# The token product as seven block products over sums of its operands

## The reference

```
x = attention(q, k, v)                     # [2, 768, 512]
theta = x @ w_theta
zr, zi = x * cos(theta), x * sin(theta)
y = w_tok_r @ zr + w_tok_i @ zi            # over the 768 tokens, both batches
u = x + y
v = u + relu(u @ w_ch)
h = relu(v @ w_in)                         # [.., 1024]
out = (h * sigmoid(conv3(h))) @ w_out
```

## Time and profile before

| | |
|---|---|
| median of 3 runs | 413.3 us (412.4 to 413.7) |
| the profiled execution's time | 412.85 us |
| its span, first to last instruction | 411.1 us |
| TensorE busy | 404.7 us (98%) |
| VectorE, ScalarE, GpSimd busy | 214.4, 215.9, 129.9 us |
| granted TensorE clock | 1.00 in all forty slices |
| moved by DMA | 32.17 MB |

### The profile page before, as it was taken

One profiled execution on the slowest core, in us unless ns is written; L12 is line 12 of the kernel. 1 busy time (PEld: TensorE's weight loads), 2 busy tenths in 40 slices (PEclk: granted clock), 3 DMA queues, 4 the chain that ended last, 5 costly groups with the idle time before them and its releaser, 6 DMA issues.

```text
span 411.1 us, 6208 instructions
## 1 busy us (share of the span) xinstructions
PE 404.7 (98%) x2268; PEld 349.0 (85%) x2268; DVE 214.4 (52%) x577; ACT 215.9 (53%) x414; POOL 129.9 (32%) x106
## 2 busy tenths in 40 slices
PE   7999999999999999999999999999999999999996
PEld 3888888888788788888898888999999898999985
DVE  5866666665788734537453251477543443434320
ACT  3766666674778546564342320378563635544431
POOL 2293000000266722248412410147653221212120
PEclk9999999999999999999999999999999999999999
DMA  7954442340000322333530000202100200010022
GB/s 253 416 217 158 159 143 93 82 153 4 0 1 2 102 78 77 85 141 125 186 129 1 2 0 0 104 0 53 51 2 0 78 1 1 16 63 2 0 77 77
DMA packets 12271, 32.17 MB, mean 78 GB/s; under 512 B 4176, under 2 KB 4432, under 8 KB 12240
## 3 DMA queue, kind: packets, MB, share of 16 engines
q1 hardware_dynamic: 12240, 31.77, 22.6%
HBM read 28.62 MB, written 3.15 MB: 77 GB/s over the span
## 4 chain that ended last, share of the span: by engine, by line
PE 95%; DVE 2%; issue 2%; ACT 1%; ACTq 0%
PE bank L452 30%; PE bank L591 24%; PE bank L649 16%; PE bank L498 9%; PE bank L470 6%; PE bank L483 6%; PE bank L605 1%; PE bank L562 1%; PE bank L509 1%; DVE xT L1022 0%; ACT trig L776 0%; DVE bank L1030 0%; DVE trig L1129 0%; ACT xT L725 0%; ACT trig L772 0%
## 5 line engine op out<-in xcount | busy, mean ns | idle before, releaser
L591 PE MATMUL bank<-z,wT 128*128 128x512 f32 x432 | 99.3, 390 | 0.0
L591 PEld LDWEIGHTS bank<-z,wT 128*128 128x128 f32 x432 | 80.8, 188 | 16.6
L452 PE MATMUL bank<-vT,win 128*128 128x386 f32 x384 | 73.3, 340 | 0.0
L452 PEld LDWEIGHTS bank<-vT,win 128*128 128x128 f32 x384 | 68.4, 188 | 1.8
L649 PE MATMUL bank<-wout,g 128*128 128x512 f32 x288 | 69.6, 390 | 0.0
L649 PEld LDWEIGHTS bank<-wout,g 128*128 128x128 f32 x288 | 53.9, 188 | 9.7
L1206 DVE SCALAR_TENSOR_TENSOR bank<-h_sb,convw,bank 128x384 f32<-128x384 f32 x32 | 19.9, 623 | 66.7 <-ACT bank L865 66.7
L859 ACT ACTIVATE h_sb<-bank 128x386 f32<-128x386 f32 x32 | 15.8, 494 | 74.0 <-PE bank L452 72.9
L414 POOL TENSOR_TENSOR g<-gf,g 128x384 fp32r<-128x384 f32 x32 | 32.5, 1017 | 68.0 <-ACT g L879 68.0
L498 PE MATMUL bank<-v_sb,pT 128*128 128x65 f32 x352 | 44.6, 268 | 0.0
L498 PEld LDWEIGHTS bank<-v_sb,pT 128*128 128x128 f32 x352 | 43.1, 192 | 0.0
(11 more groups left out here) (77 smaller groups left out, 501.8 us busy)
## 6 DMA issues: line engine op xcount, KB each, us to landing
wrows<-w_tok_laid SPq DMA_DIRECT2D x12, 768.0 KB, 4.4
v_sb<-v_laid SPq DMA_DIRECT2D x8, 780.0 KB, 4.6
qk_sb<-qk_laid SPq DMA_DIRECT2D x7, 792.0 KB, 4.3
out<-ob SPq DMA_DIRECT2D x12, 256.0 KB, 2.2
winraw<-w_in_in SPq DMA_DIRECT2D x4, 512.0 KB, 3.8
woutraw<-w_out_in SPq DMA_DIRECT2D x8, 256.0 KB, 2.7
wthraw<-w_theta_in SPq DMA_DIRECT2D x1, 1024.0 KB, 12.1
wchraw<-w_ch_in SPq DMA_DIRECT2D x1, 1024.0 KB, 5.1
```

What stands on the lines that cost most here:

```text
L452: last = pe.matmul(dst, w[a], m[b], start=(i == 0 and j == 0), stop=(i == n - 1 and j == 2))
L591: last = pe.matmul(Y_BANK[s % 2][:], wT[s % 2][:, hi, ri * NT + blk, :], z[b][:, blk, lo, ri, :], start=(blk == 0 and ri == 0 and j == 0), ...
```

## The change

The product y = [Wr Wi] [zr; zi] for both batches at once is a 2 x 2 block product: the rows of W in two halves of 384, the contraction in the real and the imaginary half (768 each), the columns in two batches of 512. It is now computed by seven block products in place of eight. A block product k is three row tiles i, so s = 3k + i runs from 0 to 20, with 18 matmuls each. The left operands are sums or differences of four blocks of W, the right ones of zr and zi of the two batches (`B_RAW`), and each result is added to or subtracted from one or two chunks of x (`ADDS`).

- Left operands: during attention GpSimd (`prepare`) forms them from the raw weights. Six (k = 0 and 1) stay in SBUF, fifteen go by four staging tiles to DRAM (`store_a`) and come back before their product (`load_a`). Nine of these are stored unsplit and split on return (`high_a` on ScalarE, `low_a` on VectorE, 768 elements). The two buffers of values (v) of attention become three, so that v of a pair is loaded earlier.
- Right operands: z is kept unsplit. `high_b`/`low_b` split one operand of 6 blocks into one of two buffers, in three pieces of 1024 elements. Six differences (three of batch 0, three mixed) are made by VectorE (`own_difference`, `other_difference`), nine sums by GpSimd (`sums`, `last_sums`), 1024 elements each.
- The first block product fills three banks at once, block by block of z, the second the next three; later ones use two banks.
- `add_y` has two VectorE additions for k < 5, one for k = 5 and 6.
- `high_u` writes a second, unrounded copy of u, with which `add_mix` is one VectorE operation in place of two.
- The chunks are finished in the order 1, 2, 0, 3, and the orders of all engines follow that. Loads of w_in and w_out come later.

In the lists of ScalarE and VectorE the lines of the old order that have no part in the new one are left out below.

```diff
--- before.py
+++ after.py
...
+        a_ops = at("a_ops", [P, 6, 2, NT, P], F32R, 41)
...
+        NI = NT // 2
+        NS = 7 * NI
+        NK = 5 * NI
+        ADDS = (((1, ALU.add), (3, ALU.subtract)), ((1, ALU.add), (0, ALU.add)), ((2, ALU.add), (0, ALU.subtract)),
+                ((2, ALU.add), (3, ALU.add)), ((0, ALU.add), (3, ALU.add)), ((0, ALU.add),), ((3, ALU.add),))
+        B_RAW = (zi[0], zi[1], zd, zr[0], zi[0], zr[1])
+        MIXED = (1, 2, 0, 3)
+        U_DONE = (2 * NI, 4 * NI, 6 * NI, 7 * NI)
+
+        def y_bank(s):
+            return bank[(6, 7, 4, 5, 0, 1)[s]] if s < 2 * NI else bank[6 + s % 2]
+
+        def b_side(k):
+            return (k + 1) % 2
...
             def load_v(p):
...
+                if p >= 3:
+                    sp.wait_ge(o_ready, NT * (p - 2))
+                sp.dma_start(v_of[p % 3], v_laid[p]).then_inc(v_in[p % 3], 16)
+
+            def load_w_raw(i):
+                if i >= 2:
+                    sp.wait_ge(staged, 5 * (i - 1))
+                for half in range(2):
+                    sp.dma_start(w_raw[:, i % 2, half].rearrange("p r n -> p (r n)"),
+                                 w_tok[i + NI * half].rearrange("p n c -> p (n c)")).then_inc(w_raw_in[i % 2], 16)
+
+            def store_a(m):
+                i, part = divmod(m, 5)
+                sp.wait_ge(staged, m + 1)
+                whole = slice(0, 2) if part < 2 else slice(0, 1)
+                sp.dma_start(a_kept[NI * part + i][:, whole], stage[m % 4][:, whole].bitcast(F32)).then_inc(stored_a[m % 4], 16)
 
             def banded():
-                for p in range(2, NP):
-                    if p + 1 < NP:
-                        load_qk(p + 1)
+                kept = 0
+                for p, count in zip(range(3, NP), (0, 5, 1, 4, 5)):
+                    load_qk(p)
                     load_v(p)
+                    for m in range(kept, kept + count):
+                        store_a(m)
+                        if m == 4:
+                            load_w_raw(2)
+                    kept += count
...
+            def load_a(n):
+                if n == 0:
+                    for m in range(4):
+                        sp.wait_ge(stored_a[m], 16 * ((NK + 3 - m) // 4))
+                sp.wait_ge(y_ready, n + 1 if n < 4 else n + 3)
...
+            def prepare(i):
+                (w_r0, w_i0), (w_r1, w_i1) = ([w_raw[:, i % 2, half, ri] for ri in range(2)] for half in range(2))
+                pool.wait_ge(w_raw_in[i % 2], 32 * (i // 2 + 1))
+                steps = 7 * i
+
+                def step(ins):
+                    nonlocal steps
+                    ins.then_inc(prep_step, 1)
+                    steps += 1
+                    pool.wait_ge(prep_step, steps)
+
+                def whole(dst, a):
+                    step(pool.tensor_copy(dst[0], a))
+                    return pool.tensor_tensor(dst[1], a, dst[0].bitcast(F32), ALU.subtract)
+
+                def summed(dst, a, b, op):
+                    step(pool.tensor_tensor(w_sum[:], a, b, op))
+                    return whole(dst, w_sum[:])
+
+                def kept(part):
+                    m = 5 * i + part
+                    if m >= 4:
+                        pool.wait_ge(stored_a[m % 4], 16 * (m // 4))
...
+                    return [stage[m % 4][:, half] for half in range(2)]
+
+                def resident(slot):
+                    return [a_ops[:, slot, half].rearrange("p n c -> p (n c)") for half in range(2)]
+
+                if i:
+                    pool.wait_ge(staged, 5 * i)
+                step(summed(resident(i), w_r1, w_i1, ALU.add))
+                whole(resident(NI + i), w_i1)
+                summed(kept(0), w_r0, w_i0, ALU.add).then_inc(staged, 1)
+                whole(kept(1), w_r0).then_inc(staged, 1)
+                for part, a, b, op in ((2, w_r0, w_i1, ALU.add), (3, w_i0, w_i1, ALU.subtract), (4, w_r1, w_r0, ALU.subtract)):
+                    pool.tensor_tensor(kept(part)[0].bitcast(F32), a, b, op).then_inc(staged, 1)
 
             def banded():
                 pool.wait_ge(bias_ready, H)
+                prepare(0)
+                prepare(1)
                 split_w_theta()
-                for s in range(2):
-                    split_rows(s)
+                prepare(2)
...
+            def sums(two):
+                blks = slice(2 * two, 2 * two + 2)
+                for dst, a in ((zr[1], zr[0]), (zr[0], zi[1])):
+                    pool.tensor_tensor(dst[:, blks, :], a[:, blks, :], dst[:, blks, :], ALU.add).then_inc(sum_ready, 1)
+
+            def last_sums(two):
+                blks = slice(2 * two, 2 * two + 2)
+                pool.wait_ge(sum_ready, 2 * two + 2)
+                pool.tensor_tensor(zi[0][:, blks, :], zr[0][:, blks, :], zi[0][:, blks, :], ALU.add).then_inc(sum_ready, 1)
+
+            pool.wait_ge(z_lo, NT)
+            pool.wait_ge(t_ready, NI)
+            sums(0)
+            sums(1)
+            low_v(0)
+            low_v(1)
+            sums(2)
+            low_v(2)
+            pool.wait_ge(b_lo, NI)
+            for two in range(NI):
+                last_sums(two)
+            for n in range(3, 2 * CB):
+                low_v(n)
...
+            def first_tokens():
+                pe.wait_ge(x_done, NU)
+                pe.wait_ge(staged, NK)
+                for blk in range(NT):
+                    pe.wait_ge(z_lo, blk + 1)
+                    for i in range(NI):
+                        for j, (hi, lo) in enumerate(((0, 0), (0, 1), (1, 0))):
+                            last = pe.matmul(y_bank(i)[:], a_ops[:, i, hi, blk, :], b_ops[:, b_side(0), blk, lo, :],
+                                             start=(blk == 0 and j == 0), stop=(blk == NT - 1 and j == 2))
+                        if blk == NT - 1:
+                            last.then_inc(y_ready, 1)
+
             def mix_tokens(s):
...
+                k, i = divmod(s, NI)
+                side, slot = b_side(k), a_slot(s)
+                if k >= 2:
+                    n = s - 2 * NI
+                    if n < 2 * NI:
+                        pe.wait_ge(a_in[n % 4], 16 * (n // 4 + 1))
+                    else:
+                        pe.wait_ge(a_lo, n - 2 * NI + 1)
+                    pe.wait_ge(u_ready, n + 1 if n < 2 else s - 1)
+                for blk in range(NT):
+                    if k >= 1 and i == 0 and blk % 2 == 0:
+                        pe.wait_ge(b_lo, NI * (k - 1) + blk // 2 + 1)
+                    for j, (hi, lo) in enumerate(((0, 0), (0, 1), (1, 0))):
+                        last = pe.matmul(y_bank(s)[:], a_ops[:, slot, hi, blk, :], b_ops[:, side, blk, lo, :],
+                                         start=(blk == 0 and j == 0), stop=(blk == NT - 1 and j == 2))
+                last.then_inc(y_ready, 1)
...
+            first_tokens()
+            for s in range(NI, 2 * NI + 1):
                 mix_tokens(s)
             transpose_u(0)
-            mix_tokens(6)
+            mix_tokens(7)
             mix_channels(0, 0)
             mix_channels(0, 1)
-            mix_tokens(7)
+            mix_tokens(8)
             mix_channels(0, 2)
             mix_channels(0, 3)
+            for s in range(9, 13):
+                mix_tokens(s)
             transpose_u(1)
-            mix_tokens(8)
+            mix_tokens(13)
             mix_channels(1, 0)
             mix_channels(1, 1)
-            mix_tokens(9)
+            mix_tokens(14)
             mix_channels(1, 2)
             mix_channels(1, 3)
+            for s in range(15, 19):
+                mix_tokens(s)
             transpose_u(2)
-            mix_tokens(10)
-            mix_tokens(11)
-            mix_channels(2, 0)
+            mix_tokens(19)
+            for j in range(CB):
+                mix_channels(2, j)
+            mix_tokens(20)
             hidden(0)
-            mix_channels(2, 1)
             transpose_u(3, (0, 1))
             hidden(1)
-            mix_channels(2, 2)
+            transpose_u(3, (2, 3))
             hidden(2)
-            mix_channels(2, 3)
             hidden(3)
-            hidden(4)
-            transpose_u(3, (2, 3))
-            for j in range(CB):
-                hidden(5 + j)
-                mix_channels(3, j)
+            mix_channels(3, 0)
+            mix_channels(3, 1)
+            mix_channels(3, 2)
+            mix_channels(3, 3)
+            for n in range(4, FB + 1):
+                hidden(n)
...
+                if t == 0:
+                    act.wait_ge(staged, NK)
+                    for m in range(4):
+                        act.wait_ge(stored_a[m], 16 * ((NK + 3 - m) // 4))
...
+            def high_b(k):
+                if k >= 2:
+                    act.wait_ge(y_ready, NI * (k - 1))
+                if k == 2:
+                    act.wait_ge(zf_ready, TT)
+                if k == 3:
+                    act.wait_ge(t_ready, NI)
+                if k == 4:
+                    act.wait_ge(sum_ready, 2 * NI)
```

(134 more changed lines are left out.)

315 lines of the change are left out of this document (128 added, 187 removed).

## The result

The changed kernel takes 416.18 us (median of 5 runs, 415.18 to 416.95) against 413.02 (5 runs, 412.4 to 413.7): ratio 1.0074, 95% interval 1.0053 to 1.0095. It is slower by 0.7%. The time lies inside the range and on the wrong side: 412.2 was forecast, with 0.52 for faster. The range held it only because it reached into the case of the falling clock, which had a chance of 0.10.

What follows compares the result with a forecast made beforehand. TensorE, busy for 98% of the span, was taken to bound the kernel. 412.85 - 12.3 (matmuls) - 0.5 (theta) + 12.2 (new waits) = 412.25, forecast 412.2 us, range 405 to 417.5.

Steps and rivals of the forecast that it cites:

- the case of the falling clock: Rival: TensorE's clock falls to 1.2 GHz behind new token-product gaps, net some +5, 417 us; chance 0.10 including a longer backlog.
- -12.3 for 54 matmuls: Token product: 432 matmuls become 378 at 0.228 us each, saving 12.3 us; called the certain part.
- Attention, cost 0: Attention: GpSimd's weight preparation ends near 83 us with slack about 14 us, so nothing reaches TensorE; cost 0.
- Theta, -0.5: Theta stage: splitting z over 512 columns, not 1024, removes a VectorE delay on the chain: -0.5 us (bounds 0 and -1.3).
- How the engines hold each other up: Token product: two-SBUF-input VectorE passes and GpSimd passes exclude each other and alternate, subtractions about 3.3 us; chance 0.62 with the walk's waits.
- VectorE keeps the ports: Rival, token product: VectorE's back-to-back passes hold off a waiting GpSimd; waits 8.1 us, 408.2 us; chance 0.20.
- little of it is felt: Rival, token product: own differences uncontested, sums mostly in VectorE's gaps; waits 3 to 4 us, 403.5 us; chance 0.08.
- The walk: Queues followed by durations around the token product and hidden stage: TensorE waits summing to 12.6 us, taken as 12.2.
- The step that failed: Token product: TensorE's clock taken as 1.00 in the main case, so waits of 2.8 and 4.4 us bring no slowdown.
- the 1.2 forecast ahead of (1,0): After product 12, channel product (1,0) waits for VectorE's low_u(1), at 217.4 against 216.2: 1.2 us.
- the hidden stage, 0.9: Hidden products without channel products between them: two banks absorb most of the 2.97 us step, cost 0.9 us (bounds 0 and 7.8).
- the race of `low_b(4,0)`: At 193.5 us, whether VectorE's low_b(4,0) or GpSimd's sum starts first hangs on 0.15 us, worth 0.8 at product 12.

Runs made afterwards that it cites:

- e7_fill_late: Changed kernel with 17 matmuls that nobody reads filling TensorE's wait ahead of product 12 only: 414.14 us, ratio 1.0039.
- e1_fill: Changed kernel with three TensorE waits of the token product filled by matmuls that nobody reads (12, 4 and 17): 414.49 us, ratio 1.004.
- e6_order3: Changed kernel with VectorE reordered in three parts, the last moving three add_y ahead of low_b(2) and add_mix(12) ahead of hidden 3's convolution: 406.7 us, ratio 0.9858.
- The first two new orders: Changed kernel with VectorE's order altered so additions precede held-up subtractions: first part 412.71 us, second part on top of it 409.14 us.
- the third: Same run as e6_order3, on top of the first two new orders: 406.7 us, ratio 0.9858.
- e4_hidden: Changed kernel with the last four channel products put between hidden products 3 to 8 again, other engines' orders matched: 418.16 us, ratio 1.0124.
- e3_order: Changed kernel, VectorE reordered: add_mix(0), add_mix(1) between the low_b(3); low_a(6), add_y(10) ahead of low_b(4,1), low_b(4,2): 412.71 us, ratio 0.9988.
- e9_halves: e6_order3 with each of GpSimd's nine block sums done as two passes of 512 elements in place of one of 1024: 408.87 us, ratio 0.9888.

## Why the prediction was right and wrong

- **-12.3 for 54 matmuls: right.** L701 and L681 issue 378, and a product takes 4.12 us.
- **Attention, cost 0: right, with a miss on the way.** GpSimd began at 21.9 (it waited for its weights, not for the bias) and ended at 90.6, not 83, 11 us ahead of `turns(0)`, which waits for it. TensorE issued 84 and 83 matmuls in the windows of the earlier trace rows.
- **Theta, -0.5: not shown.** By the same timeline product 0 started at 137.19 in before, at 137.11 in after and at 136.31 to 137.48 in the other profiled runs, which have the same theta stage; that spread is larger than the term.
- **How the engines hold each other up: right.** Alternation pass by pass, 3.3 us a subtraction, is what the timelines show; "VectorE keeps the ports" (408.2) fell at once with the 9.69 us, and "little of it is felt" with it.
- **The walk: right to 0.3 us.** I had `add_mix(0)` end at 184.4, product 12 start at 206.7; the trace has 184.6 and 206.73. The single waits differ (none ahead of product 11, where I had 1.4), because the slow clock had made products 9 and 10 late, and that is the same time put elsewhere: e7_fill_late, where the clock stayed up there, has 1.1 ahead of product 11.
- **The step that failed: that TensorE runs at full clock behind the new waits.** I had taken 1.00 from a trace without such waits, and gave the fall of the clock, with its backlog, 0.10. It fell behind both. What it cost is less than the two slow stretches are long (1.6 and 2.5 us): the first is swallowed by the wait for product 12, the second took the place of the 1.2 forecast ahead of (1,0). The runs put the whole at 1.4 to 1.7 (e1_fill). My "one product each, up to +8, net +5" in the rival was too large in every part but had the place right. It is not enough for the wrong side: e1_fill, with the clock at 1.00, is at 1.004 where the forecast was at 0.9985 of the kernel before, 2.3 us more; the next term and the 0.9 below it make 2.5.
- **The term that was mis-sized: the hidden stage, 0.9.** From hidden product 0 to the first output product it took 31.17 us for 28.7 of matmuls, so 2.5. What it has over the forecast is `add_mix(12)`, which stood behind the convolution of hidden 3. e6_order3 moved it, and the stage took 29.69 us, so 1.0 over the matmuls, close to my 0.9. My walk had put the table load and the copies of u there and not this place in VectorE's order.

From 410.5 (the forecast in terms of the span) to 414.7: +0.9 until product 12 (the theta gain and 0.4 for the race of `low_b(4,0)`, neither of which came), +2.5 for the slow product 12, -1.2 for the wait that it replaced, +1.6 in the hidden stage; 0.4 is left, some 0.02 in each product and 0.15 behind the first output. The chances were wrong as a whole: with the likeliest case at the bound of "same", a term that could only lengthen (the clock) was kept out of it and put in a rival of its own, though the walk itself forecast the waits of 2.8 and 4.4 us.

On the clock, the Trainium skill's rule (page "TensorE: Matmul & The Clock Gate", "Part 1: The HAM clock gate"), that it follows how busy the engine has lately been and has two levels, agrees with the windows at 0.61 and 0.71 behind the waits and with 1.00 once they were filled. On the ports, the Trainium skill's rule (page "SBUF — State Buffer", "SBUF: two separate sides"), that of a VectorE operation with two SBUF inputs and a GpSimd one the first gets the shared ports for its whole instruction, agrees with 3.2 us a subtraction beside the sums and 1.2 without.

## What to carry to other kernels

Where TensorE is the bound, taking work from it is worth only what the engines that feed it can follow. Walk their queues by durations, and count a wait of 2.5 us or more twice, once for itself and once for the clock behind it (it fell behind seven of the nine such waits in these traces and behind none of 2.0 or less), unless a later wait swallows that. Two-SBUF-operand passes of VectorE beside a row of GpSimd passes take their own time plus the rest of the running one: put nothing that TensorE waits for behind them. The first two new orders, which do that, were worth some 7 us, a part of it the clock, and the third, which moves work out of the way of later waits, 2 more, without removing a single instruction. And ask of an order that looks worse what load it hides before undoing it.

## What was not expected of the hardware

The clock did not fall behind every wait of the same length. Behind the wait of 2.6 us ahead of (0,2) it fell in after, and stayed at 1.00 in the profiled runs of e4_hidden (2.60) and e7_fill_late (2.58); behind 2.54 in e3_order and 2.55 in e4_hidden it fell; behind 3.5 to 4.0 it fell each time (four traces), and behind 2.0 and less never. What tells the like cases apart is open. The five runs of the changed kernel spread over 1.8 us, and the time goes with the clock: 415.2 us at a mean of 0.996, 415.7 at 0.992, 416.2 to 417.0 at 0.988. The executions of e7_fill_late and of e9_halves divide in the same way.

Cutting GpSimd's passes in halves lengthened its three last sums from 8.8 to 12.1 us beside VectorE's subtractions. That fits turns taken pass by pass, in which an engine with twice as many passes gives way more often; no run tests it further. Some 0.5 us of it is the halves themselves: a GpSimd pass of 512 alone takes 1.29 us, one of 1024 2.4.
